# Attention with V one turn behind the transposes of P, later quotients, and four places for V

## The reference

```
# attention, by chunks of 32 queries; 16 keys before, 8 after, 8 memory keys ahead of them
k_full = concat(mem_k, k[l_start:r_end]);  v_full = concat(mem_v, v[l_start:r_end])
s = scale * q_c @ k_full.T;  a = exp(s - max(s));  a = a / (sum(a) + 1e-9);  out_c = a @ v_full
# gated product, x is 3072 x 512, hidden 1536
x = ((x @ w_a) * (x @ w_b)) @ w_out
# 8 experts, hidden 1024, every token through every expert, weighted by a Sinkhorn gate
P = 8 rounds of row and column normalization of exp(x @ w_gate - max)
out += P[:, e] * (relu(x @ w1[e]) @ w2[e])   for e in 0..7
```

## Time and profile before

| what | value |
|---|---|
| median of 3 runs | 2624.56 us (2621.55 to 2624.56) |
| time of the profiled execution | 2619.76 us |
| its span, first to last instruction | 2618.0 us |
| PE busy | 2554.0 us (98%) |
| PE busy in the first 160 us | 122.6 us |
| granted PE clock, mean | 0.995 of full speed |

### The profile page before, as it was taken

One profiled execution on the slowest core, in us unless ns is written; L12 is line 12 of the kernel. 1 busy time (PEld: TensorE's weight loads), 2 busy tenths in 40 slices (PEclk: granted clock), 3 DMA queues, 4 the chain that ended last, 5 costly groups with the idle time before them and its releaser, 6 DMA issues.

```text
span 2618.0 us, 38013 instructions
## 1 busy us (share of the span) xinstructions
PE 2554.0 (98%) x14418; PEld 2103.1 (80%) x14418; DVE 1559.1 (60%) x2293; ACT 994.5 (38%) x1722; POOL 1640.6 (63%) x1329
## 2 busy tenths in 40 slices
PE   7889999999999999999999999999999999999998
PEld 6678878788778888888888888888887888888887
DVE  3555544544667555555566666666666566666666
ACT  4653322322434334343343333333334433333333
POOL 2385400200477777777767777877779777777776
PEclk8999999999999999999999999999999999999999
DMA  9765544334266666666665554555554555555553
GB/s 208 161 223 221 211 151 161 148 145 149 104 257 230 255 252 230 235 257 251 249 242 208 204 226 177 217 193 188 214 189 187 211 209 205 197 201 209 187 223 117
DMA packets 190061, 530.42 MB, mean 203 GB/s; under 512 B 55544, under 2 KB 124088, under 8 KB 170680
## 3 DMA queue, kind: packets, MB, share of 16 engines
q1 hardware_dynamic: 168792, 517.43, 53.7%
q10 hardware_dynamic: 21088, 10.55, 1.6%
HBM read 367.41 MB, written 160.60 MB: 202 GB/s over the span
## 4 chain that ended last, share of the span: by engine, by line
PE 92%; DVE 3%; issue 2%; POOL 2%; ACT 2%; ACTq 0%; DVEq 0%; POOLq 0%
PE bank L1010 46%; PE bank L1109 22%; PE bank L1087 19%; PE bank L918 1%; PE bank L972 1%; PE bank L948 1%; DVE tmp L1734 1%; POOL H L871 1%; PE bank L960 1%; POOL X L749 0%; PE bank L982 0%; ACT X L1346 0%; DVE hid L1888 0%; DVE hid L1944 0%; PE bank L987 0%
## 5 line engine op out<-in xcount | busy, mean ns | idle before, releaser
L1010 PE MATMUL bank<-X,W 128*128 128x512 f32 x5550 | 1397.1, 390 | 11.7 <-DVE tmp L1731 4.2
L1010 PEld LDWEIGHTS bank<-X,W 128*128 128x128 f32 x5550 | 1038.5, 188 | 236.4 <-issue 17.3
L871 POOL TENSOR_TENSOR H<-tmp,H 128x512 fp32r<-128x512 f32 x448 | 579.6, 1307 | 285.5 <-ACT H L1550 284.3
L1109 PE MATMUL bank<-H,W2n 128*128 128x512 f32 x2688 | 682.3, 389 | 5.6 <-POOL H L871 2.4
L1789 DVE TENSOR_TENSOR Y<-Y,bank 128x512 f32<-128x512 f32 x752 | 496.9, 682 | 262.4 <-PE bank L1109 262.3
L1109 PEld LDWEIGHTS bank<-H,W2n 128*128 128x128 f32 x2688 | 504.1, 188 | 112.9 <-POOL H L871 6.3
L1550 ACT ACTIVATE H<-tmp 128x512 fp32r<-128x512 f32 x448 | 276.9, 630 | 464.9 <-DVE tmp L1819 238.8
L1087 PE MATMUL bank<-W,hid 128*128 128x512 f32 x1536 | 385.5, 390 | 2.6 <-DVE Y L1769 1.5
L1087 PEld LDWEIGHTS bank<-W,hid 128*128 128x128 f32 x1536 | 287.9, 188 | 64.2 <-issue 4.2
L749 POOL TENSOR_TENSOR X<-Y,X 128x1024 fp32r<-128x1024 f32 x30 | 79.8, 2667 | 368.5 <-ACT X L1346 368.5
L1766 DVE SCALAR_TENSOR_TENSOR Y<-bank,gate,Y 128x512 f32<-128x512 f32 x224 | 167.0, 747 | 165.8 <-PE bank L1087 164.7
(11 more groups left out here) (121 smaller groups left out, 2140.3 us busy)
## 6 DMA issues: line engine op xcount, KB each, us to landing
W<-w_kept SPq DMA_DIRECT2D x88, 1792.0 KB, 11.6
W2n<-w2n_kept SPq DMA_DIRECT2D x64, 1536.0 KB, 8.2
w_kept<-W SPq DMA_DIRECT2D x44, 1792.0 KB, 8.1
raw<-in_moe_w_dram SPq DMA_DIRECT2D x64, 512.0 KB, 4.3
w2n_kept<-W SPq DMA_DIRECT2D x32, 1024.0 KB, 7.9
w2n_kept<-tmp SPq DMA_DIRECT2D x64, 512.0 KB, 7.9
W2n<-w2n_kept SPq DMA_DIRECT2D x64, 256.0 KB, 3.2
W<-w_kept SPq DMA_DIRECT2D x12, 1024.0 KB, 9.1
```

Of the source, the lines that this page charges most:

```text
L871: nc.gpsimd.tensor_tensor(H[:, pos, 1], hidden_at(k, pos), H[:, pos, 0].bitcast(F32), ALU.subtract).then_inc(h_lo, 1)
L1010: last = nc.tensor.matmul(into[:, :], W1[:, c % 2, ws, w_slot, kc, :], X[:, pos, xs, kc, :], start=(start and kc == 0 and n == 0), stop=(k ...
L1109: last = nc.tensor.matmul(b_half[pair][half][:, :], W2n[k % 2][:, a, blk, half * P:(half + 1) * P], H[:, h, b, :], start=(q in (0, 5) and ...
```

## The change

Three things are altered together. On PE, weigh_v moves to the turn after next (weigh_v(r-2) in turn r, directly behind scores(r)), transpose_p(r-1) comes behind it and the first unit, and transpose_o moves to r-3; what falls out of the loop at its end, weigh_v(22) and transpose_o(21), stands ahead of up(0,0). On ACT x_quad goes to r-3 and behind exps(r). On DVE quotients go to r-2, with two places for the reciprocals. V gets four places, and with them `g < VS` in load_v lets two more DMAs of `mem_v` rows through in the fourth turn of each batch; load_v(3) moves ahead of put_rows(1) to put_rows(3). Small tiles move to another part of memory, and three waits ahead of the first W2 follow them.

```diff
-    VS = 3
+    VS = 4
...
-            return sum((12, 10, 10, 8, 8, 10)[i % G] for i in range(r % VS, r + 1, VS))
+            return sum((12, 10, 10, 10, 8, 10)[i % G] for i in range(r % VS, r + 1, VS))
...
             load_v(2)
+            load_v(3)
             for b in range(1, B):
                 put_rows(b)
...                      # POOL, down_lo(0)
-                    pool.wait_ge(a_on, 2 * R)
+                    pool.wait_ge(a_sum, R)
...                      # PE
                 scores(r)
-                if r > 0:
-                    transpose_p(r - 1)
                 if r > 1:
-                    transpose_o(r - 2)
+                    weigh_v(r - 2)
                 for unit in QUAD_UNITS[r][:1]:
                     transposed(unit)
                 if r > 0:
-                    weigh_v(r - 1)
+                    transpose_p(r - 1)
+                if r > 2:
+                    transpose_o(r - 3)
                 for unit in QUAD_UNITS[r][1:]:
                     transposed(unit)
...
+            weigh_v(R - 2)
+            transpose_o(R - 3)
             pe.wait_ge(a_sub, 2 * R)
             up(0, 0, 0)
...                      # ACT, down_hi(0)
-                    act.wait_ge(a_sum, R)
+                    act.wait_ge(a_o, R)
...
                     copy_pt(r - 1)
-                if r > 1:
-                    x_quad(r - 2)
                 exps(r)
+                if r > 2:
+                    x_quad(r - 3)
...
+            x_quad(R - 3)
             copy_pt(R - 1)
...                      # DVE; rsum is now [P, 2, HP, 2]
                     denominators(r - 1)
-                    quotients(r - 1)
+                if r > 1:
+                    quotients(r - 2)
...
             denominators(R - 1)
+            quotients(R - 2)
             quotients(R - 1)
```

More of the change, by code:

```diff
@@ L132, in build @@
             PT = sb("PT", [P, HP, P], F32, first)
-            On = sb("On", [P, HP, 2, HD], F32, first)
             Df = sb("Df", [P, HP, 2, KEYS], F32, first)
             Pr = sb("Pr", [P, 2, HP, 2, KEYS], F32, first)
-            nmax = sb("nmax", [P, 2, HP], F32, first)
-            esum = sb("esum", [P, HP, 2, 2], F32, first)
-            rsum = sb("rsum", [P, HP, 2], F32, first)
         hid0 = sb("hid0", [P, 2, 2, 2, TB], F32R)
@@ L144, in build @@
             KT1 = sb("KT1", [P, HP, KCOLS], F32, first)
+            On = sb("On", [P, HP, 2, HD], F32, first)
+            nmax = sb("nmax", [P, 2, HP], F32, first)
+            esum = sb("esum", [P, HP, 2, 2], F32, first)
+            rsum = sb("rsum", [P, 2, HP, 2], F32, first)
         hid1 = sb("hid1", [P, 2, 2, 2, TB], F32R)
@@ L1321, in down_hi @@
                 if w == 0:
-                    act.wait_ge(a_pt, R)
-                    act.wait_ge(a_sum, R)
+                    act.wait_ge(a_o, R)
                 elif w >= 2:
@@ L1648, in denominators @@
                 dve.wait_ge(a_sum, r + 1)
-                nc.vector.tensor_reduce(rsum[:, :, :], esum[:, :, :, :], AX.X, ALU.add).then_inc(a_den, 1)
+                nc.vector.tensor_reduce(rsum[:, r % 2], esum[:, :, :, :], AX.X, ALU.add).then_inc(a_den, 1)
                 dve.wait_ge(a_den, r + 2)
-                nc.vector.reciprocal(rsum[:, :, :], rsum[:, :, :]).then_inc(a_rs, 1)
+                nc.vector.reciprocal(rsum[:, r % 2], rsum[:, r % 2]).then_inc(a_rs, 1)
             def quotients(r):
@@ L1661, in quotients @@
                                             b_o[f][:, 0:HP * HD].rearrange("p (j n) -> p j n", j=HP),
-                                            rsum[:, :, f:f + 1].to_broadcast([P, HP, HD]),
+                                            rsum[:, r % 2, :, f:f + 1].to_broadcast([P, HP, HD]),
                                             ALU.mult).then_inc(a_on, 1)
```

## The result

The changed kernel takes 2629.16 us (median of 18 runs, 2626.09 to 2634.68); the kernel before, on the same chip, 2621.97 (18 runs, 2615.75 to 2625.62). The ratio is 1.0027, with a 95% interval of 1.0020 to 1.0034: slower by 0.27%, about 7.2 us, and beyond what a measurement can take for no change. The forecast of 2628.5 lies beside that number and its range holds it. But it was added up as 4.0 us on a median of 2624.56, and the loss is 7.2 us on a median that measured 2.6 us lower here; and the loss did not come from where the forecast put it.

The account below looks back on a forecast made before the run. It took SP's queue issuing V to bound the end of attention; 3.0 us for eight added DMAs plus 1.0 us of clock made 4.0 us on a median of 2624.56, taken as 2628.5, range 2621.5 to 2632.

Parts of the forecast that it names:

- The stage: End of attention, weigh_v(23): the loss arises there, and the stage behind it shifts by the same amount.
- V in four places: SP's queue: eight more DMAs of memory rows ahead of V(23) cost 3.0 us, bounds near zero and 4.6.
- Where it lands: End of attention: V(23) lands at 153.0 instead of 150.0, so weigh_v(23) starts 3.0 us later.
- a sign against it: SP's queue: SP waiting for a place would show the forecast wrong; it expected no pause.
- ACT, DVE, POOL: Attention turns: transpose_p 1.2 us later, exps and an operand's copy about 0.8; free while V is late, otherwise 0.8.
- The sum for DVE: DVE per turn without units: 3.5 us of work, less than the 3.6 to 4.2 of a turn now.
- The clock: Between 144 and 153 us, at the new V waits: one fall to half clock costs 1.0 us, bounds 0 and 3.4.
- A: weigh_v's waits vanish, PE gets up to 7.2 us back: faster, 2617 to 2620; chance 0.10.
- The share of it in which the holes would go as well: PE's holes inside groups: a new order removes them too, some of 19.3 us on top; no separate chance.
- B: PE and SP share the pace of instruction loads; vanished waits return as holes: no change, 2624 to 2626; chance 0.22.
- C: Turns 22 and 23: clock falls a second time at the V waits, 6.4 us slower, 2631; chance 0.25.
- the four: The forecast, chance 0.43, and rivals A, 0.10, B, 0.22, and C, 0.25.

Follow-up runs that it names:

- e1: Changed kernel with PE, ACT and DVE in the order of the kernel before; V's four places, eight extra DMAs and moved tiles stay: 1.0008 of the kernel before.
- e10: Changed kernel with two places for PT, nothing else altered: 1.0028 of the kernel before.
- e5: Changed kernel with each step on PE and ACT in its old place of the turn, only the one-turn lag kept: 1.0039 of the kernel before.
- e9: e5 with two places for PT: 1.0005 of the kernel before.
- e2: Changed kernel with transpose_p(r-1) directly behind scores(r) and weigh_v(r-2) behind the first unit: 1.0017 of the kernel before.
- e3: Changed kernel with quotients(r-2) ahead of denominators(r-1) on DVE: 1.0030 of the kernel before.
- e6: e5 with up(0,0) ahead of weigh_v(22) and operand_lo(0,0,3) behind quotients(21): 1.0032 of the kernel before.
- e7: Changed kernel run once more without any edit: 1.0028 of the kernel before.
- e12: e1 with the memory rows of put_rows(1) to put_rows(3) issued through ACT's queue: 1.0003 of the kernel before.
- e4: Changed kernel with x_quad(r-3) behind the units' copies on ACT: 1.0024 of the kernel before.
- e8: Kernel before with memory rows of batches 1 to 3 issued from ACT's queue in place of SP's: 0.9997 of the kernel before.

## Why the prediction was right or wrong

*The stage: right.* The two traces differ by 12.9 us at the end of weigh_v(23) and by 14.9 at the end of the span; what follows attention shifted by it, and the 2.0 us more are not explained.

*The steps "V in four places" and "Where it lands": wrong for this kernel.* They said that V's queue delays weigh_v(21), (22) and (23), by 3.0 us. No weigh_v waited for V there, and SP paused 3.7 us for a place, which the forecast itself named as a sign against it. Alone (e1) the eight DMAs delayed no V that the trace shows; weigh_v(23) starts 0.1 us later. The error was to price a queue by its median hold when a third of its time, 47.7 of 137 us, was in holds of 0.8 us or more; of the 27 such holds from 20 us on, 22 begin within 0.5 us of one of PE's instruction packets. e1 timed at 0.08%, with an interval that holds both zero and 3.0 us, so the price itself is not settled; that it was not what made the changed kernel slow is (no wait for V).

*The step "ACT, DVE, POOL": this one failed.* It saw that transpose_p comes 1.2 us later in its turn, and exps and the copy of an operand with it, and wrote "It costs nothing while V is late, and 0.8 if V is not". Three things were left out. The delay was sized as the work of weigh_v and one unit, and is 1.9 us on average over the turns (3.1 from scores to transpose_p against 1.2), since a hole, a unit or half clock can fall between. It was weighed only for the turns without units, and the loss came in turns 14 to 17, where the K and Q copies behind exps hold PE up. And V's lateness covers nothing there, because it acts from turn 21 on. That PT has one place stood ahead of the forecast and in none of its steps; in the changed order it is hidden behind PE's own order (e10), but with the old places it costs the whole loss by itself (e5 against e9: 0.39 to 0.05%). So two things each push copy_pt back, PE's order and the single PT, and taking one away is not enough while the other is there: slower by 0.28% with two places and the late transposes (e10), by 0.17 and 0.39% with one place and the early ones (e2, e5), by 0.05% with neither (e9).

*The sum for DVE, "3.5 us", "less than the 3.6 to 4.2 of a turn now": wrong in one turn.* With operand_lo(0,0,3) in it, turn 22 of DVE takes 5.0 us without a pause, PE's 4.2, and weigh_v(22) waits 2.83 us. e3 and e6 bought nothing measurable by shortening it, so its part in the 7.2 us is small or comes back as holes; the runs do not tell which.

*The clock: the sign right, the place too narrow.* The forecast had one fall between 144 and 153 us, for 1.0 us. The trace has 44.4 us at half clock (1.2 GHz) in attention instead of 23.9, e7 37.5. Near the end it falls in the wait for quotients at weigh_v(22), not behind one for V, and six matmuls take 2.10 us there instead of 1.66. Half clock adds to the loss in this kernel, but the loss does not need it: e6, slower by 0.32%, has no more of it than the kernel before.

*The rivals.* A (the waits vanish, faster) had its condition fulfilled: in e12 they did vanish, and it brought nothing. The share of it in which the holes would go as well is answered by e5 and e6, with about 15 us of holes and no gain. B's mechanism, a common pace of instruction loads, is what e1 and e12 agree with; its number was too low, because something else made the loss. C's number, 2631, is 1.8 us off, the forecast's 0.7, but in the changed kernel no V wait stood ahead of its clock. None of the four had the true cause: a stage delayed on ACT. That 2628.5 met 2629.16 is luck: neither of its two terms, V's 3.0 us and the clock behind V's waits, is what happened, and the change, 7.2 us against 4.0, met the number only because the kernel before measured 2.6 us lower than the median that the forecast started from.

*Left open.* The holes sum to 20.7 us before (16; the forecast's 15, and one of 1.44 us at the head of a unit) and 30.2 in the changed kernel (20), 28.9 in e7; but 14.5 in e5, which is no faster. They do not explain the loss by themselves; what sets their length was not found. Nor do the summed waits give the size of the loss kernel by kernel: e4 has 12.0 us for 0.24%, e2 14.6 for 0.17%.

## What to carry to other kernels

When a stage is moved a turn back, count the places of every tile that it reads or that is rewritten in that turn, not only of the one whose load was late: V got its place and P's transposed copy did not. Then ask of each in-order engine what stands behind the instruction that is now released later; behind ACT's copy stood the exponentials and the copies that PE's next steps need, and there a delay of 1 to 2 us a turn became a loss. And before spending on a wait at the head of a group, look whether its time would reappear: removing all waits for V (e12) moved the kernel by nothing that could be measured.

## What the runs showed of the hardware

PE's holes inside groups fall on a fixed instruction number. Counting PE's weight loads, matmuls and semaphore instructions, each lies at number 193 past a multiple of 256, in every profiled kernel, whatever instruction stands there. The instruction queue's 116 packets carry 1.90 MB, 16 KB each; the trace has 29656 such instructions of PE, 256 for a packet. In attention, where 256 instructions took as little as 3.5 us in the kernel before, 16 of 28 such points have a hole in the kernel before, 20 of 28 in the changed one, up to 4.4 us long. The Trainium skill, "Runtime: NRT & Kernel Launch", section "Instruction fetch mechanics", says that blocks of 256 instructions are fetched while the current one executes, so that the fetch is mostly hidden. The block agrees with the trace; that it is hidden does not, with 16 holes and 20.7 us before.

Long holds of SP begin at such moments: in the kernel before two of 1.3 us at 134.56 and 142.50 us, PE's instruction packets at 134.60 and 142.44. From 100 to 148 us it has 12 such packets, and at 11 of them a hold of 0.9 us or more begins within 0.5 us; it has no other hold of that length there. It suggests that SP, issuing V, and PE, loading instructions, are slowed by one thing, which no run separated; adding or taking away DMAs on SP (e1, e8, e12) changed the time by 0.08% or less, within the intervals.
